# Moving transposes, weight splits and copies by one place in the hand-written schedule of a spectral mixer and a feed-forward layer

## The reference, cut to what matters

```python
# x is 4 x 3008 x 256
X = np.fft.rfft(x, axis=1)                       # Xr, Xi
Yr = Xr @ w_r - Xi @ w_i + b_r                   # weights 256 x 256
Yi = Xr @ w_i + Xi @ w_r + b_i
Y  = soft_threshold(Yr, 0.01) + 1j * soft_threshold(Yi, 0.01)
y  = np.fft.irfft(Y, n=3008, axis=1).reshape(12032, 256)
h  = y @ w_in                                    # 256 x 2048
g  = np.maximum(h, 0) + alpha * np.minimum(h, 0) # alpha: one slope per hidden unit
out = g @ w_out                                  # 2048 x 256
```

## Time and profile before

| | |
|---|---|
| median of 3 runs | 1379.79 us (1379.56 to 1382.8) |
| the profiled execution | 1382.8 us, of which the span from the first to the last instruction is 1381.0 us |
| granted TensorE clock, mean | 0.997 |
| busy: PE, DVE, ACT, POOL | 98%, 74%, 55%, 23% |
| head of the kernel | to 114 us |
| a tile without transform work | 46 us |

### The profile page before, as it was taken

How to read it: one execution, slowest core, us unless ns; L and a number is a source line. 1 busy time by engine, 2 the same in 40 slices (tenths; PEclk the granted TensorE clock), 3 DMA queues, 4 the chain that set the end, 5 groups by cost and what they waited for, 6 DMA issues and landing times.

```text
span 1381.0 us, 21709 instructions
## 1 busy us (share of the span) xinstructions
PE 1359.8 (98%) x6921; PEld 1156.8 (84%) x6921; DVE 1022.4 (74%) x1890; ACT 765.4 (55%) x1710; POOL 319.5 (23%) x361
## 2 busy tenths in 40 slices
PE   7999999999999999999999999999999999999997
PEld 4987888888888888888888888888888888888886
DVE  6786688898866768989876667888886566566654
ACT  4775566665544555666644545666564444444443
POOL 1443533332201422333200332323220000000000
PEclk9999999999999999999999999999999999999999
DMA  7644533232211542323212243233311121102101
GB/s 256 180 144 152 166 77 85 70 90 66 54 44 37 149 119 60 85 68 86 65 43 48 80 115 86 67 79 78 87 43 41 28 50 39 25 26 50 27 16 16
DMA packets 174676, 106.83 MB, mean 77 GB/s; under 512 B 112198, under 2 KB 150366, under 8 KB 174563
## 3 DMA queue, kind: packets, MB, share of 16 engines
q1 hardware_dynamic: 170412, 101.60, 27.4%
q10 hardware_dynamic: 3959, 3.70, 0.8%
q0 software_dynamic: 192, 0.15, 0.1%
HBM read 67.88 MB, written 37.49 MB: 76 GB/s over the span
## 4 chain that ended last, share of the span: by engine, by line
PE 92%; DVE 2%; DMA 2%; ACT 2%; issue 1%; POOL 1%; SPq 0%; ACTq 0%; POOLq 0%; DVEq 0%
PE out_ps L558 39%; PE h_ps L558 38%; PE work_ps L558 11%; PE work_ps L658 2%; PE work_ps L592 2%; PE work_ps L660 1%; PE work_ps L593 1%; DMA fwd_scratch<-g_raw 1%; ACT above L878 0%; DVE shrunk L1114 0%; DMA table<-in_twiddles_dram 0%; PE h_ps L733 0%; DMA inv_scratch<-inv_sb 0%; ACT shr_hi L884 0%; DVE x_lo L1044 0%
## 5 line engine op out<-in xcount | busy, mean ns | idle before, releaser
L914 ACT ACTIVATE rows<-h_ps 128x502 f32<-128x502 f32 (+1 forms) x384 | 225.7, 588 | 510.1 <-PE h_ps L558 510.1
L1145 DVE SCALAR_TENSOR_TENSOR g_raw<-rows,keep,h_ps 128x502 f32<-128x502 f32 (+1 forms) x384 | 280.2, 732 | 267.2 <-ACT rows L914 264.0
L558 PE MATMUL out_ps<-g_hi,wout_hi 128*128 128x502 f32 (+1 forms) x768 | 305.0, 397 | 0.1
L558 PE MATMUL h_ps<-y_hi,win_hi 128*128 128x502 f32 (+1 forms) x768 | 299.8, 390 | 0.3 <-DVE g_raw L1145 0.3
L558 PE MATMUL out_ps<-g_hi,wout_lo 128*128 128x502 f32 (+1 forms) x768 | 299.8, 390 | 0.0
L558 PE MATMUL h_ps<-y_lo,win_hi 128*128 128x502 f32 (+1 forms) x768 | 299.7, 390 | 0.0
L558 PE MATMUL out_ps<-g_lo,wout_hi 128*128 128x502 f32 (+1 forms) x768 | 299.0, 389 | 0.0
L558 PE MATMUL h_ps<-y_hi,win_lo 128*128 128x502 f32 (+1 forms) x768 | 298.8, 389 | 0.0
L1044 DVE TENSOR_TENSOR g_lo<-g_raw,g_hi 128x502 fp32r<-128x502 f32 (+2 forms) x385 | 267.8, 695 | 1.8 <-ACT g_hi L923 1.4
L923 ACT ACTIVATE g_hi<-g_raw 128x502 fp32r<-128x502 f32 (+1 forms) x384 | 237.1, 617 | 6.6 <-DVE g_raw L1145 6.2
L558 PEld LDWEIGHTS h_ps<-y_hi,win_hi 128*128 128x128 f32 x768 | 145.0, 189 | 31.0 <-issue 0.7
(11 more groups left out here) (159 smaller groups left out, 2013.4 us busy)
## 6 DMA issues: line engine op xcount, KB each, us to landing
pair_raw<-fwd_scratch SPq DMA_DIRECT2D x96, 128.0 KB, 2.2
rows<-inv_scratch SPq DMA_DIRECT2D x61, 192.0 KB, 2.4
table<-in_twiddles_dram SPq DMA_DIRECT2D x28, 384.0 KB, 3.4
inv_scratch<-inv_sb SPq DMA_DIRECT2D x36, 256.0 KB, 2.2
x_raw<-in_x_dram SPq DMA_DIRECT2D x56, 160.0 KB
fwd_scratch<-staging SPq DMA_DIRECT2D x46, 192.0 KB, 2.1
inv_sb<-inv_scratch SPq DMA_DIRECT2D x122, 64.0 KB, 2.4
out_dram<-turned SPq DMA_DIRECT2D x124, 40.0 KB, 1.8
```

The costliest lines, as they stand in the source:

```text
L558: mm = pe.matmul(ps, lhs, rhs, start=(first and n == 0), stop=(last and n == len(terms) - 1), **kw)
L914: act.activation(negpart[:, q % 2, 0:size], h_ps[:, q % 2, 0:size], ACT.Relu, scale=-1.0).then_inc(negpart_done, 1)
L1145: dve.scalar_tensor_tensor(g_raw[:, q % 2, 0:size], negpart[:, q % 2, 0:size], keep[:, m:m + 1], h_ps[:, q % 2, 0:size], ALU.mult, ALU.add ...
```

## The change

Three things move. In `turn`'s step on DVE the order was transpose half 0, rest of step 0, transpose half 1, bend of step 1; it becomes transpose half 0, bend of step 1, rest of step 0, transpose half 1. In tile 0 the splits of weight chunks 2 to 7 go from steps 1, 3, 5, 7, 9, 11 to steps 0, 2, 4, 6, 8, 10, on ACT, DVE and POOL, and `split_back` and `rest_back` of the second and third pair of rows from steps 6 and 10 to 5 and 9, as in the other tiles. In tile 1 the split of the mixing weights goes from steps 3 and 4 to steps 1 and 2.

```diff
 def i_split(f, m):
-    if f == 0 or m <= 2:
-        return i_bpair(f, m - 2)
-    return i_bpair(f, m - 1)
-
-def ffw_unit(f, m):
-    w = (m + 3) // 2
-    return w if f == 0 and m % 2 == 1 and w < CHUNKS else None
+    return i_bpair(f, 0) if m == 2 else i_bpair(f, m - 1) if m > 2 else None
...
-                    if f == 1 and m in (3, 4):
-                        split_mixw(m - 2)
+                    if f == 1 and m in (1, 2):
+                        split_mixw(m)
...
-                    w = ffw_unit(f, m)
-                    if w is not None:
-                        split_ffw(w)
+                    if f == 0 and m % 2 == 0 and m // 2 + 2 < CHUNKS:
+                        split_ffw(m // 2 + 2)
...
+                    if f >= 1 and m == LAG - 1:
+                        turn(f - 1, 0)
                     q = f * STEPS + m
-                    turning = f >= 1 and m == LAG - 1
-                    if turning:
-                        turn(f - 1, 0)
-                    if turning or q in ALONE:
+                    if q in ALONE:
                         rest_bent(*divmod(q - 1, STEPS))
-                    if turning:
-                        turn(f - 1, 1)
                     bend(f, m)
                     p = p_unit(f, m, 0)
                     if p is not None:
                         whole_spec(p)
-                    if q >= 1 and not turning and q not in ALONE:
+                    if q >= 1 and q not in ALONE:
                         rest_bent(*divmod(q - 1, STEPS))
+                    if f >= 1 and m == LAG - 1:
+                        turn(f - 1, 1)
...
-                    if f == 1 and m in (3, 4):
-                        rest_mixw(m - 2)
+                    if f == 1 and m in (1, 2):
+                        rest_mixw(m)
```

More of the change, by code:

```diff
@@ L1291, in _ @@
                         rest_whole(p)
-                    w = ffw_unit(f, m)
-                    if w is not None:
-                        rest_win(w)
+                    if f == 0 and m % 2 == 0 and m // 2 + 2 < CHUNKS:
+                        rest_win(m // 2 + 2)
                     p = p_couple(f, m, 3)
@@ L1405, in _ @@
                         rest_sum(p)
-                    w = ffw_unit(f, m)
-                    if w is not None:
-                        rest_wout(w)
+                    if f == 0 and m % 2 == 0 and m // 2 + 2 < CHUNKS:
+                        rest_wout(m // 2 + 2)
                     if s_unit(f, m + 2) is not None:
```

## The result

The changed kernel takes 1387.70 us (median of 6, 1387.29 to 1390.43), the kernel before 1379.99 (median of 6). The ratio is 1.0062, with a 95% interval of 1.0051 to 1.0074: slower, as forecast, and by 7.7 us instead of 5.7 (the ratio, which also takes in further runs of both kernels, is worth 8.6 us). On the 1379.79 that the prediction started from, this ratio is 1388.3, 0.1 above its range.

A forecast was written before the change was run, and what follows sets the result against it. PE, busy for 98% of the span, was taken as the bound, each new wait paid in full. Turns and tile 1 (5.4 us) plus tile 0 (0.3) gave 5.7 us on 1379.79, so 1385.5 us; range 1382.4 to 1388.2.

The forecast's parts named there:

- The turn: Turns of 14 tiles: the bend ahead of the rest makes PE wait 0.24, 0.40 or 0.27 us each.
- Tile 1: Turn of tile 1: the rest waits for POOL's moved mixing-weight subtraction, so PE loses 1.24 us.
- The extra 0.10 for the late load: Each late handoff to PE: the matmul after the late one comes 0.10 us later than usual.
- Rival 4: Late handoffs to PE: no extra 0.10 us, so 4.2 us slower in all, 1384.0; chance 0.13.
- Tile 0: Moved splits in the first tile: +0.3 us net, with rests in even steps having about 2 us of margin.
- the early rows: Tile 0, `split_back` in steps 5 and 9 before its rows land: taken as 0, upper end 0.4 us each.
- The 0.89 at 119: Tile 0, first rest: held up by POOL's part of weight chunk 2, so PE loses 0.89 us.
- the 0.56 to be won: Tile 0: PE's waits of 0.11 us at 121.80 and 0.45 us at 128.08 go away.
- A growth of tile 0 by more than 1 us: Sign named in advance that the prediction is wrong: the first tile grows by over 1 us.
- 1 (the port effect fails): Tiles 0 and 1: POOL does not hold up DVE's rest, so 3.8 us slower in all, 1383.6; chance 0.15.
- 2 (the turn hides the bend): Turns: the bend holds DVE under 0.37 us, PE never waits, not slower, 1379.2; chance 0.10.
- 3 (tile 0 jams): Tile 0: fuller even steps or early `split_back` add two or three waits of 0.4 to 1 us, about 1388; chance 0.12.

The follow-up runs named there:

- pool_held: The changed kernel, with POOL's parts of weight chunk 2 and the mixing weights held until the DVE rest each had met is done; 1387.38 us, ratio 1.0041.
- mixw_only: The kernel before, with only the mixing weights' split moved to steps 1 and 2 of tile 1; one execution, tile 1 53.17 us.
- filler_192: The kernel before, plus one DVE instruction of 0.25 us between first transposes and rest in each of the 23 turns; 1380.31 us, ratio 0.9998.
- pool_held_4: The changed kernel, with POOL's parts of weight chunks 2 and 3 and the mixing weights held until DVE rests are done, run again; 1387.52 us, ratio 1.0048.
- pool_held_2: The changed kernel, with POOL's parts of weight chunks 2 and 3 and the mixing weights held until DVE rests are done; 1390.40 us, ratio 1.0063.
- turn_only: The kernel before, with only the new order of the turn on DVE; 1385.93 us, ratio 1.0037.

## Why the prediction was right or wrong

- *The bound.* Right behind the head: PE has no slack there, and every new wait was paid in full. The reading of the clock was too coarse. A 9 in a slice stands for 90% or more, and the profiled execution had the clock at 0.50 from 48.1 to 51.5 us. Its head takes 114.35 us, and 111.8 to 112.8 in the executions without such a stretch; that can account for most of the 3.0 us by which it lay above the median. The forecast is a difference, so it doesn't hang on this.
- *The sum.* By tiles it is 7.8 us for 5.7. The first tile was forecast 1.3 us too small, the turns of 14 tiles 1.1 too small.
- *The turn.* Right in mechanism, place and count: 15 turns, the waits named `g_lo`, nothing in the seven other tiles apart from tile 12's chance. The terms were too small: 0.24, 0.40 and 0.27 were 0.30, 0.44 (with the chance of tile 20 once 0.66) and 0.33. Behind the bend the rest takes 0.67 us and not the 0.64 that it takes behind transposes, and 0.02 to 0.03 came on top of the starts. Over 14 turns that is 5.28 against 4.2, of which 0.2 is the chance of tile 20.
- *Tile 1.* Right: 1.24 forecast, 1.17 measured, and `pool_held` and `mixw_only` show the meeting of the two moves.
- *The extra 0.10 for the late load.* Right. The Trainium skill's rule on weight loads (TensorE: Matmul & The Clock Gate, Step-by-step: what each phase is for) does not take it away: the load starts with the matmul at 506.56, and the next matmul comes after 0.33. Rival 4 falls.
- *Tile 0.* This is the step that failed: "rests have about 2 us of margin there, so nothing", and for the early rows "I take 0". The term was +0.3 and measured 1.64. The 0.89 at 119 (0.84) and the 0.56 to be won were right. Missing were 0.79 at 125.6 and 0.62 at 155. No row showed the 2 us. In the trace of before the rest was 1.9 to 2.4 us ahead of PE in steps 3 to 9, but 0.71 in step 2 and 1.42 in step 10, and these are the two further steps at which PE now waits. I had counted DVE's and ACT's work in the even steps, but not applied to DVE's other subtractions the effect that I had just used for the rest. Now `rest_win` and `rest_first` stand in the same step as `rest_wout` on POOL, the second one starts inside POOL's operation and takes 1.68 us (1.11 in the kernel before, 0.69 alone). With the 0.84 lost ahead, the rest of step 2 starts 11.28 us into the tile, where it started at 9.23. A growth of tile 0 by more than 1 us was named as a sign that the prediction is wrong, and it came. The early rows, kept as an upper end of 0.4 each, cost 0.5 in this company and 4.6 alone.
- *The rivals.* 1 (the port effect fails) and 2 (the turn hides the bend) fell; `filler_192` shows that 2 would have held for an instruction of 0.25 us. 3 (tile 0 jams) is what came on top, with two waits of 0.6 to 0.8 us, at a chance of 0.12. The forecast's own mechanism and this rival do not exclude each other, and I had priced them as if they did: 5.7 + 1.4 would have been near the 7.7.

What stays open: why a rest takes 0.03 us more behind a bend, why some tiles take 0.2 us more in small steps, when the clock of the head falls, and which of the meetings of DVE and POOL between steps 2 and 10 of `pool_held_4` starts its late chain.

## What to carry to other kernels

Where one engine is busy all the time, ask of every reordering what the other engines hand to it next and by how much they are early: here 0.25 us were free where a half has two transposes, 0.44 cost 0.10, and 0.61 cost 0.31. The order of a queue is worth nothing by itself; it is worth the margin of the last thing that the full engine waits for. Two moves that are free alone can meet: when DVE and POOL both read SBUF, 0.3 us (in one place 0.03) decide which of the two waits for the other, so check each moved POOL operation against every DVE operation of its step, not only the one on the path.

## What the runs showed of the hardware

- A DVE subtraction of two SBUF operands that starts inside a POOL operation ends 0.53 to 0.56 us behind its end, with 502 columns on 128 partitions as with 512 on 32, though alone they take 0.68 and 0.69. The rounding of x, with one operand in SBUF, is held up too and ends 0.28 behind (in the kernel before 1.50 us from 126.81, POOL from 126.30 to 128.03; alone 0.42). The bend, with one operand in PSUM, is not (0.74 us from 120.12 in the kernel before, inside POOL's operation from 119.76 to 121.21).
- With starts 0.03 us apart or less it goes either way: at 124.17 in the kernel before DVE was not held up and POOL's operation took 2.17 us, at 122.4 in `filler_192` POOL took 1.30 and DVE 1.54.
- One instruction of 0.44 us on DVE cost 0.7 us in a tile with over 1 us of margin, because it let POOL start first.
- In `pool_held_2` the granted TensorE clock was at full (2.4 GHz) until 108.7 us, at 0.50 (1.2 GHz) until 118.9, and at full again behind; its head takes 115.9 us. PE had been busy for 7.48 of 8.60 us from 100 us on. A stretch of 3.4 us at 0.50 in the head is in 8 of the 16 profiled executions, of both kernels. Before the one of the kernel before PE was busy for 5.59 of 7.00 us from 40 us on; in `turn_only`, which has none, for 5.46 of the same 7.
